# First of two expert mixtures: three passes of fp32r parts for fp32 products, with the weights split by GpSimd and the rows gathered ahead

## The chip, the cores and the metric

One core of one Trainium2 chip. The metric is the device time of one execution in microseconds (us), the median of several runs. The engines are TensorE (PE; its weight loads are shown as PEld), VectorE (DVE), ScalarE (ACT), GpSimd (POOL) and SyncE (SP), which here only issues DMAs.

## What is computed

```python
kv = einsum('bhsd,bhse->bhde', k, v); out = einsum('bhsd,bhde->bhse', q, kv)   # 8 x 8 x 576 x 64
x = out / rms(out) * g_norm                       # as 4608 rows of 512
# first mixture: every row goes to one expert of 8
e_idx = argmax(x @ w_gate); gate_w = softmax(x @ w_gate)[e_idx]; eom = sigmoid(x @ w_output_gate)[e_idx]
for e in range(8):                                # w1[e]: 512 x 1024, w2[e]: 1024 x 512
    out[e_idx == e] = gate_w * eom * (relu(x[e_idx == e] @ w1[e]) @ w2[e])
# second mixture: all pairs (row, expert) by falling score; a row takes the first expert that has
# room (576 rows each), then relu(x @ w21[e]) @ w22[e]
```

Everything is fp32, inputs and output.

## The kernel before

**Attention.** A hand-interleaved schedule over 8 batches of 6 chunks. GpSimd multiplies the rows by the inverse root (L492) and stores them to the DRAM tensor `x_rows`, three chunks at a time (L498).

**Routing.** VectorE finds each row's expert and its slot in a list sorted by expert, in which each expert fills whole tiles of 128 rows (L1040 to L1115); TensorE adds the one-hot lists up (L623). The semaphore `s_route` (L1115) says that `tok_i`, the row numbers of each tile, is there. `T1` = 43 is the greatest count of tiles; on this input the eight experts fill 5, 5, 6, 5, 5, 4, 6 and 5 tiles, and the last two are padding.

**First mixture**, the part that changes. For each tile t:

- GpSimd copies the tile's row numbers (L513), then gathers 128 rows of 520 numbers (512 and the row's factor) into the one buffer `xg` (L516), when the rows before have been turned.
- TensorE, in one step of its loop: the first product of tile t (L633: two halves of 512 columns, four chunks each), the turning of tile t+1's rows (L672, four transposes), the second product of tile t-1 (L686, eight chunks), the turning of tile t's h (L693, eight transposes). An fp32 matmul shows as two records, so a product is 16 records.
- VectorE copies the turned rows and the turned h out of PSUM (L1127, L1132), and scores y of tile t-2 against the second router: eight operations with an accumulator (L1138), one for each expert, `y` times a row of `wg2b`, written to `prod`.
- ScalarE does relu (L855) and the scaling of y by the factor (L863), and issues the store of y to `y_rows`.
- SP loads an expert's weights, 4 MB, into one of two sets when the second product of the expert before the preceding one is done (L410, L411).

The loops are real loops with registers; the set of weights is picked by a register read from `tile_par`.

**Selection and second mixture.** VectorE and TensorE search the thresholds of each expert (L1246, L739), and TensorE works through 40 tiles in three passes of fp32r parts: high times high, low part of the weights times high part of the rows, high times low (L648 in `in_parts`). ScalarE makes the high parts with plain copies (L878, L893, L900), VectorE the low parts by subtraction (L1171, L1177, L1184). None of this changes.

```python
passes = ((acts[0], w[0]), (acts[0], w[1]), (acts[1], w[0]))      # 0: high, 1: low
for i in range(3 * chunks):
    a, b = passes[i // chunks]
    if i == 2 * chunks:
        pe.wait_ge(*low_x)                                        # low part of the rows
    mm = pe.matmul(ps, a[:, i % chunks, :], b[:, i % chunks, cols], ...)
```

Of the kernel before, what the change touches and what calls it, by code (L numbers as in the profile page):

```python
# [30 lines left out]
P = 128  # L31
# [28 lines left out]
def build(nc, q, k, v, g_norm, w_gate, w_og, w1, w2, w_gate2, w21, w22, out, debug=None):  # L60
# [20 lines left out]
    HALF = F // 2  # L81

# [26 lines left out]
    with ExitStack() as ctx:  # L109
# [17 lines left out]
        wg2_rows = nc.dram_tensor("wg2_rows", [1, E, DM], F32, kind="Internal").ap()  # L127
        y_rows = nc.dram_tensor("y_rows", [T1 * P, DM], F32, kind="Internal").ap()
# [38 lines left out]
        gcur = sb("gcur", [P, 1], I32)  # L167
# [42 lines left out]
        s_gc = sem("gather_index")  # L210
        s_xg = sem("rows_gathered")
# [8 lines left out]
        s_yst = sem("y_stored")  # L220
# [25 lines left out]
        with ExitStack() as early:  # L246
            def sbe(name, shape, dt=F32):
                return early.enter_context(nc.sbuf_tensor(name, shape, dt))

            xrow = [sbe(f"xrow{i}", [PT, CT, DM]) for i in range(2)]  # L250
            lgs = sbe("lgs", [PT, G1, 2 * E])
# [6 lines left out]
            kvgb = [sbe(f"kvgb{i}", [P, HP, P + 4 * E]) for i in range(2)]  # L258
            kvT = sbe("kvT", [P, HP, P])
            qT = [sbe(f"qT{i}", [P, HP, PT]) for i in range(2)]  # L260
            sq = [sbe(f"sq{i}", [PT, DM]) for i in range(2)]
            q2 = [sbe(f"q2{i}", [PT, DM]) for i in range(2)]
            lraw = [sbe(f"lraw{i}", [PT, CT, H * 2 * E]) for i in range(2)]
        with ExitStack() as router:
            wg2b = router.enter_context(nc.sbuf_tensor("wg2b", [P, E, DM], F32))
            prod = router.enter_context(nc.sbuf_tensor("prod", [P, E, DM], F32))
            router.enter_context(nc.sbuf_tensor("room_of_routing", [P, 2048], F32))
            wg2_t = router.enter_context(nc.sbuf_tensor("wg2_t", [E, DM], F32))
# [23 lines left out]
        w1_sb = w_sb[:, :, 0:KC * F].rearrange("p u (c f) -> p u c f", c=KC)  # L292
        w2_sb = w_sb[:, :, KC * F:].rearrange("p u (c f) -> p u c f", c=FC)
# [36 lines left out]

        ohb = sb("ohb", [P, T1, P], F16)
        bid = sb("bid", [P, T1, P], F16)
        cmp = sb("cmp", [P, T1, NTH], F16)
        room_n = sb("room_n", [P, P], F16)
        ind = sb("ind", [P, NTH], F16)
        best = sb("best", [P, T1])
        a3 = sb("a3", [P, T1, E])
        b3 = sb("b3", [P, T1, E])
        taken = sb("taken", [P, T1, E])
# [30 lines left out]
        ty_ps = bank[6]  # L370
        l8_ps = bank[7]
# [21 lines left out]

        @block.sync
        def _(sp):
# [13 lines left out]
            def load_weights(n, u, w1_src, w2_src):  # L409
                sp.dma_start(w1_sb[:, u, :, :], w1_src.rearrange("(p c) f -> p c f", c=KC)).then_inc(s_wl, 16)  # L410
                sp.dma_start(w2_sb[:, u, :, :], w2_src.rearrange("(p c) f -> p c f", c=FC)).then_inc(s_wl, 16)  # L411
                sp.wait_ge(s_wl, (n + 1) * 32)
                alone(sp)

            load_weights(0, 0, w1[0], w2[0])
            sp.wait_ge(s_fa, 1)
            load_weights(1, 1, w1[1], w2[1])
            sp.wait_ge(s_route, 1)
            with sp.Fori(1, E // 2) as j:
                for u in range(2):  # L420
                    e = j * 2 + u
                    end = sp.value_load(ends_i[0:1, bass.ds(e - 2, 1)], min_val=1, max_val=T1 + 1)
                    sp.wait_ge(s_l2, end)
                    alone(sp)
                    load_weights(e, u, w1[e], w2[e])
# [30 lines left out]
        def _(pool):  # L456
# [45 lines left out]
            pool.wait_ge(s_fa, 1)  # L502
            for b in range(B):
                pool.dma_start(x_rows[b * S:(b + 1) * S, DM:XW].rearrange("(p c) n -> p c n", c=CT),
                               fac[:, b * CT:(b + 1) * CT, :]).then_inc(s_fst, 16)
            pool.wait_ge(s_wgc, 1)
            pool.dma_start(wg2_rows[0, :, :], wg2_t[:, :]).then_inc(s_wgs, 16)
            pool.wait_ge(s_wgs, 16)
            pool.dma_start(wg2b[:, :, :], wg2_rows[:, :, :].to_broadcast([P, E, DM])).then_inc(s_wgb, 16)


            def gather_x(t):
                pool.tensor_copy(gcur[:, :], tok_i[:, bass.ds(t, 1)]).then_inc(s_gc, 1)  # L513
                pool.wait_ge(s_gc, t + 1)
                alone(pool)
                pool.indirect_dma_start(out=xg[:, :], out_offset=None, in_=x_rows[:, :],  # L516
# [37 lines left out]
        def _(pe):  # L554
# [73 lines left out]
            def first_product(n, w, half):  # L628

                if half == 0:  # L630
                    pe.wait_ge(s_xT, n + 1)
# [746 lines left out]
```

## Time and profile before

| | |
|---|---|
| median of 3 runs | 1592.75 us (1592.34 to 1598.07) |
| profiled execution | 1592.23 us, span 1590.4 us |
| PE busy | 1420.8 us, 89% of the span |
| DVE busy | 896.5 us, 56% |
| ACT, POOL busy | 366.1 us (23%), 236.0 us (15%) |
| chain that ended last | PE 78%, DVE 15% |

The first mixture runs from 240 to 894 us, the second from 974 to the end; between the two lies the first search. The page is one profiled execution. A busy TensorE is not TensorE at its peak, because the records of pipelined matmuls overlap and their ends are modelled; the time of a group of matmuls is read from one start to the next. The idle time of an engine that is not the bottleneck costs nothing.

### The profile page before, as it was taken

Reading aid. Unit: us, or ns where it says so; the run is one execution under the profiler, and the core shown is the slowest. Engines: PE = TensorE matmul, PEld = TensorE weight load, DVE = VectorE, ACT = ScalarE, POOL = GpSimd, SP = SyncE. Lnnn points to the kernel's source line nnn. Section 1 sums busy time; section 2 is a strip of 40 time slices with the busy share of each in tenths; the row PEclk is TensorE's granted clock in tenths of the full one; section 3 lists DMA queues with packets and bytes.
Section 4 is the critical chain, followed back from the end, with each engine's and each line's share of the span. In section 5 each row is a group of like instructions: output and inputs, shape, how many; then the busy total and the mean of one; then the engine's idle time right before and its main releaser. Section 6 shows DMA issues by size and latency. Waiting matters only on the chain.

```text
span 1590.4 us, 25626 instructions
## 1 busy us (share of the span) xinstructions
PE 1420.8 (89%) x9036; PEld 955.4 (60%) x9037; DVE 896.5 (56%) x2207; ACT 366.1 (23%) x647; POOL 236.0 (15%) x264
## 2 busy tenths in 40 slices
PE   5989519999999999999999525999999999999997
PEld 5878414444444444444444324787878777777786
DVE  1666782454554544544545566857676767676531
ACT  1655401111111111111111002242324232323331
POOL 1244431010110110101100001111111111111110
PEclk9999759999999999999999755999999999999999
DMA  9997250130313131331101021414141414141400
GB/s 220 250 269 235 60 199 27 40 139 33 145 33 139 40 132 40 139 126 53 33 33 34 14 92 42 140 31 140 32 140 32 146 29 143 32 140 34 144 31 23
DMA packets 49675, 151.13 MB, mean 95 GB/s; under 512 B 5144, under 2 KB 23784, under 8 KB 47408
## 3 DMA queue, kind: packets, MB, share of 16 engines
q1 hardware_dynamic: 30592, 95.43, 19.9%
q0 software_dynamic: 12800, 43.18, 8.6%
q10 hardware_dynamic: 6192, 11.27, 1.8%
q8 instruction: 61, 1.00, 0.3%
q14 instruction: 30, 0.25, 0.1%
HBM read 119.55 MB, written 30.31 MB: 94 GB/s over the span
## 4 chain that ended last, share of the span: by engine, by line
PE 78%; DVE 15%; issue 4%; DMA 1%; ACT 1%; SPq 0%; DVEq 0%; POOLq 0%; POOL 0%; ACTq 0%
PE bank L648 23%; PE bank L633 19%; PE bank L686 19%; PE bank L739 4%; PE bank L693 4%; PE o_ps L600 2%; PE kv_ps L566 1%; PE bank L672 1%; DMA v_sb<-in_v 1%; PE bank L679 1%; DVE lraw L1032 1%; DVE xrow L999 1%; PE qt_ps L588 1%; DVE cmp L1246 1%; DVE ms L969 1%
## 5 line engine op out<-in xcount | busy, mean ns | idle before, releaser
L633 PE MATMUL bank<-w_sb,xT 128*128 x688 | 305.1, 596 | 1.6 <-DVE xT L1127 1.2
L686 PE MATMUL bank<-w_sb,hT 128*128 x688 | 302.5, 592 | 1.0 <-DVE hT L1132 1.0
L633 PEld LDWEIGHTS bank<-w_sb,xT 128*128 128x128 f32 x688 | 128.4, 192 | 147.8 <-issue 147.8
L686 PEld LDWEIGHTS bank<-w_sb,hT 128*128 128x128 f32 x688 | 127.9, 191 | 145.7 <-issue 145.7
L1138 DVE SCALAR_TENSOR_TENSOR prod<-y,wg2b 128x512 f32<-128x512 f32 x344 | 213.7, 687 | 2.9 <-ACT y L863 2.9
L855 ACT ACTIVATE h<-bank 128x512 f32<-128x512 f32 x166 | 99.2, 598 | 489.7 <-PE bank L633 304.1
L1126 DVE COPY factor<-xg 128x1 f32 (+1 forms) x43 | 6.6, 154 | 287.0 <-PE bank L672 287.0
L531 POOL DMA_INDIRECT xg<-y_rows,gat_i x40 | 44.1, 1103 | 417.6 <-PE bank L679 217.5
L693 PEld LDWEIGHTS bank<-ident,h 128*128 128x128 f32 x664 | 85.6, 192 | 22.5 <-issue 20.2
L863 ACT ACTIVATE y<-bank,factor 128x512 f32<-128x512 f32 x43 | 29.6, 688 | 300.0 <-PE bank L686 300.0
L648 PE MATMUL bank<-w_lo,xT_hi 128*128 128x512 f32 x320 | 94.9, 407 | 0.4 <-DVE w_lo L1184 0.4
L648 PE MATMUL bank<-w_hi,xT_hi 128*128 128x512 f32 x320 | 93.4, 414 | 1.3 <-ACT xT_hi L878 0.8
L513 POOL COPY gcur<-tok_i 128x1 int32 (+1 forms) x43 | 16.4, 382 | 523.7 <-DVE xT L1127 515.6
L693 PE MATMUL bank<-ident,h 128*128 128x128 f32 x664 | 89.7, 279 | 0.2 <-ACT h L855 0.2
L648 PE MATMUL bank<-w_hi,hT_hi 128*128 128x512 f32 x320 | 88.0, 410 | 0.8 <-ACT hT_hi L893 0.8
L648 PE MATMUL bank<-w_hi,xT_lo 128*128 128x512 f32 x320 | 87.6, 395 | 0.0
L1132 DVE COPY hT<-bank 128x512 f32<-128x512 f32 x86 | 55.4, 686 | 54.9 <-PE bank L693 54.8
L648 PE MATMUL bank<-w_hi,hT_lo 128*128 128x512 f32 x320 | 83.4, 399 | 0.0
L648 PE MATMUL bank<-w_lo,hT_hi 128*128 128x512 f32 x320 | 83.3, 398 | 0.0
L739 PE MATMUL bank<-cmp,bid 128*128 128x15 f16 x2752 | 79.8, 171 | 0.0
L900 ACT ACTIVATE w_hi<-w_sb 128x1024 fp32r<-128x1024 f32 x64 | 63.9, 1054 | 63.8 <-SPq L442 63.8
L1184 DVE TENSOR_TENSOR w_lo<-w_sb,w_hi 128x1024 fp32r<-128x1024 f32 x64 | 77.6, 1219 | 0.0
(244 smaller groups left out, 1896.5 us busy)
## 6 DMA issues: line engine op xcount, KB each, us to landing
w_sb<-in_moe_w SPq DMA_DIRECT2D x16, 2048.0 KB, 12.5
w_sb<-in_moe_w SPq DMA_DIRECT2D x64, 512.0 KB
y_rows<-y ACTq DMA_DIRECT2D x43, 256.0 KB, 2.0
k_sb<-in_k SPq DMA_DIRECT2D x16, 576.0 KB, 14.8
v_sb<-in_v SPq DMA_DIRECT2D x16, 576.0 KB, 17.1
q_sb<-in_q SPq DMA_DIRECT2D x8, 1152.0 KB, 20.4
x_rows<-xrow POOLq DMA_DIRECT2D x16, 576.0 KB, 5.9
wg2b<-wg_rows POOLq DMA_DIRECT2D x1, 2048.0 KB, 7.3
```

Source lines behind the costliest of these rows:

```text
L531: pool.indirect_dma_start(out=xgs[w % 2][:, 0:DM], out_offset=None, in_=y_rows[:, :], in_offset=bass.IndirectOffsetOnAxis(ap=gat_i[:, w:w ...
L600: mm = pe.matmul(o_ps[x % 2][0:PT, hp // 2, hp % 2 * (P + 4 * E):(hp % 2 + 1) * (P + 4 * E)], qT[x % 2][:, hp, :], kvgb[e % 2][:, hp, :], ...
L633: mm = pe.matmul(h_ps[half][:, :], xT[:, c, :], w[:, c, half * HALF:(half + 1) * HALF], start=(c == 0), stop=(c == KC - 1))
L648: mm = pe.matmul(ps, a[:, i % chunks, :], b[:, i % chunks, cols], start=(i == 0), stop=(i == 3 * chunks - 1))
L686: mm = pe.matmul(y_ps[:, :], hT[:, i, :], w[:, i, :], start=(i == 0), stop=(i == FC - 1))
L693: mm = pe.transpose(th_ps[half][:, i * P:(i + 1) * P], h[:, half * 4 + i:F:FC], ident[:, :])
L739: mm = pe.matmul(cps[:, 0:NTH], bid[:, g, :], cmp[:, g, :], start=False, stop=(g == T1 - 1))
L855: act.activation(h[:, half * HALF:(half + 1) * HALF], h_ps[half][:, :], ACT.Relu).then_inc(s_h, 1)
L900: act.activation(w_hi[:, u, cols], w_sb[:, u, cols], ACT.Copy).then_inc(s_whi, 1)
L1132: dve.tensor_copy(hT[:, half * 4:(half + 1) * 4, :].rearrange("p a b -> p (a b)"), th_ps[half][:, :]).then_inc(s_hT, 1)
L1138: ch.inc(dve.scalar_tensor_tensor(out=prod[:, e, :], in0=y[:, :], scalar=1.0, in1=wg2b[:, e, :], op0=ALU.mult, op1=ALU.mult, accum_out=sc_ ...
L1184: dve.tensor_tensor(w_lo[:, u, cols], w_sb[:, u, cols], w_hi[:, u, cols].bitcast(F32), ALU.subtract).then_inc(s_wlo, 1)
```

## The change

**Products.** The first mixture uses `in_parts` too. ScalarE makes the high parts of the turned rows and of h, VectorE the low parts (`rows_low`, `hT_low`), by a subtraction of one operand in PSUM and one in SBUF. All loops over the 43 tiles are written out. The score operations write to PSUM (`prod_ps`, two banks in turn), from the third on with a wait for the one before the last.

**Weights.** Expert 0: ScalarE copies (`first_high(0)`) and GpSimd subtracts (`low_piece`), both after the x rows are stored. Expert 1: ScalarE copies after the routing, GpSimd subtracts after ten gathers. Experts 2 to 7: GpSimd does both, after all gathers. A piece is 128 x 1024, eight make an expert. SP loads them by pieces with two in flight.

**Gathers.** Tiles 0 and 1 are gathered into `xg` and `xg2`. The others go into one of three staging buffers, from there to `x_sorted` in DRAM (a store by SP), and from there into `xg` or `xg2` (a load issued by ScalarE, `sorted_in`). The index copy is gone.

**Moved.** The stores of the factor and the turned router go from GpSimd's to SP's queue, and `wg2b` is spread after the routing. `y` is double-buffered. Early buffers are laid out in another order.

```diff
 # SP
+for t in range(2, T1):
+    i, nth = t % STAGED, (t - 2) // STAGED + 1
+    sp.wait_ge(s_xs[i], nth * 16)
+    sp.dma_start(x_sorted[t * P:(t + 1) * P, :], xst[i][:, :]).then_inc(s_xo[i], 16)
+for e in range(2, E):
+    end = sp.value_load(ends_i[0:1, e - 2:e - 1], min_val=1, max_val=T1 + 1)
+    sp.wait_ge(s_l2, end)
+    for i in range(PIECES):
+        wait_pos(sp, s_pl[i % 2], ((e - 2) * (PIECES // 2) + i // 2) * 16)
+        load_piece(e % 2, i, w1[e], w2[e], s_pl[i % 2])
...
 # GpSimd
+def low_piece(u, i):
+    pool.tensor_tensor(w_lo[:, u, cols(i)], w_sb[:, u, cols(i)], w_hi[:, u, cols(i)].bitcast(F32),
+                       ALU.subtract).then_inc(s_split, 1)
...
+for i in range(PIECES):
+    pool.wait_ge(s_fhi, i + 1)
+    low_piece(0, i)
 pool.wait_ge(s_route, 1)
 pool.wait_ge(s_fst, 16 * B)
-gather_x(0)
-with pool.Fori(1, T1) as t:
-    pool.wait_ge(s_xT, t)
-    alone(pool)
+for t in range(10):
     gather_x(t)
+for i in range(PIECES):
+    pool.wait_ge(s_fhi, PIECES + i + 1)
+    low_piece(1, i)
+for t in range(10, T1):
+    gather_x(t)
+for e in range(2, E):
+    for i in range(PIECES):
+        pool.wait_ge(s_pl[i % 2], ((e - 2) * (PIECES // 2) + i // 2 + 1) * 16)
+        pool.tensor_copy(w_hi[:, e % 2, cols(i)], w_sb[:, e % 2, cols(i)]).then_inc(s_phi, 1)
+        pool.wait_ge(s_phi, (e - 2) * PIECES + i + 1)
+        low_piece(e % 2, i)
...
 # TensorE
+rows_in(0)
+for t in range(T1 + 1):
+    if t < T1:
+        w = one_set(w1_both, set_of(t))
+        need = pe.value_load(tile_wait[0:1, t:t + 1], min_val=PIECES, max_val=PIECES * E)
+        pe.wait_ge(s_split, need)
+        for half in range(2):
+            first_in_parts(t, w, half, None, nothing)
+    if t + 1 < T1:
+        rows_in(t + 1)
+    if t > 0:
+        second_in_parts(t - 1, one_set(w2_both, set_of(t - 1)), None, None, nothing)
+    if t < T1:
+        h_turned(t)
...
 # ScalarE
+first_high(0)
+act.wait_ge(s_route, 1)
+act.wait_ge(s_fst, 16 * B)
+first_high(1)
+rows_high(0)
+sorted_in(2)
+for t in range(T1 + 1):
+    if t < T1:
+        relu(t)
+    if t + 1 < T1:
+        rows_high(t + 1)
+    if t + 3 < T1:
+        sorted_in(t + 3)      # waits for s_xo and for s_xlo >= t + 2
+    if t > 0:
+        scaled(t - 1)
+    if t < T1:
+        hT_high(t)
...
 # VectorE
+factor_kept(0)
+rows_low(0)
+for t in range(T1 + 2):
+    if t == 2:
+        dve.wait_ge(s_wgb, 16)
+    if t >= 2:
+        scores(t - 2)
+    if t + 1 < T1:
+        factor_kept(t + 1)
+        rows_low(t + 1)
+    if t < T1:
+        hT_low(t)
```

## Rows read from the trace of the kernel before

**Rows 1.** The page, busy tenths and granted clock in 40 equal slices.
```profile
PE   5989519999999999999999525999999999999997
PEclk9999759999999999999999755999999999999999
```

**Rows 2.** Timeline, TensorE, a tile of the first mixture: start, us, what.
```profile
599.68 7.03 PE L633 MATMUL bank<-w_sb,xT 128*128 x16
...
607.02 7.03 PE L686 MATMUL bank<-w_sb,hT 128*128 x16
...
614.78 7.03 PE L633 MATMUL bank<-w_sb,xT 128*128 x16
```

**Rows 3.** Timeline, TensorE, a tile of the second mixture without a search.
```profile
1537.70 1.18 PE L648 MATMUL bank<-w_hi,xT_hi 128*128 128x512 f32 x4
...
1543.77 2.12 PE L648 MATMUL bank<-w_hi,hT_hi 128*128 128x512 f32 x8
...
1550.27 1.18 PE L648 MATMUL bank<-w_hi,xT_hi 128*128 128x512 f32 x4
```

**Rows 4.** Timeline, VectorE, the same tile of the first mixture.
```profile
608.13 0.68 DVE L1138 SCALAR_TENSOR_TENSOR prod<-y,wg2b 128x512 f32<-128x512 f32 x1
...
612.41 0.69 DVE L1138 SCALAR_TENSOR_TENSOR prod<-y,wg2b 128x512 f32<-128x512 f32 x1
...
614.53 1.29 DVE L1132 COPY hT<-bank 128x512 f32<-128x512 f32 x2 [1.01 <-PE bank L693]
```

**Rows 5.** Timeline, VectorE and GpSimd in attention, from several windows.
```profile
80.02 1.84 DVE L1032 TENSOR_TENSOR lraw<-lraw,rin 96x768 f32<-96x768 f32 x1
81.01 1.75 POOL L492 TENSOR_TENSOR xrow<-xrow,rin 96x512 f32<-96x512 f32 x1
...
182.67 2.05 POOL L492 TENSOR_TENSOR xrow<-xrow,rin 96x512 f32<-96x512 f32 x2
182.77 3.77 DVE L1032 TENSOR_TENSOR lraw<-lraw,rin 96x768 f32<-96x768 f32 x1
...
196.29 0.95 DVE L1032 TENSOR_TENSOR lraw<-lraw,rin 96x768 f32<-96x768 f32 x1
...
200.44 0.72 POOL L498 DMA_DIRECT2D x_rows<-xrow  x1 [0.30 <-POOL xrow L492]
```

**Rows 6.** Two lines alone: durations in ns, min/median/max, first and last start.
```profile
L492 POOL TENSOR_TENSOR xrow<-xrow,rin x48: 1032/1042/1798, 58.9 to 203.2; 96x512 f32<-96x512 f32 x48
...
L999 DVE TENSOR_TENSOR xrow<-o_ps,g_sb x48: 616/686/687, 36.5 to 192.3; 96x512 f32<-96x512 f32 x48
```

**Rows 7.** Timeline, the routing's steps and the first product.
```profile
211.92 0.55 DVE L1075 TENSOR_TENSOR inc<-inc,cnt 96x384 f32<-96x384 f32 x1
...
233.38 0.18 DVE L1115 TENSOR_SCALAR cap_v<-cap_v 128x43 f32<-128x43 f32 x1
...
240.56 9.63 PE L633 MATMUL bank<-w_sb,xT 128*128 x16 [1.24 <-DVE xT L1127]
```

**Rows 8.** ScalarE's weight copy (ns min/median/max); then DMA issues, us to landing.
```profile
L900 ACT ACTIVATE w_hi<-w_sb x64: 1039/1051/1073, 958.9 to 1519.9; 128x1024 fp32r<-128x1024 f32 x64
...
y_rows<-y ACTq DMA_DIRECT2D x43, 256.0 KB, 2.0
...
xg<-x_rows,gcur POOLq DMA_INDIRECT x43, 3.6
```

**Rows 9.** Timeline, SP's issues of weight loads (L410: first mixture, L437: second).
```profile
327.52 0.35 SPq L410 DMA_DIRECT2D w_sb<-in_moe_w  x1
...
402.98 0.34 SPq L410 DMA_DIRECT2D w_sb<-in_moe_w  x1
...
644.47 0.34 SPq L410 DMA_DIRECT2D w_sb<-in_moe_w  x1
...
704.85 0.34 SPq L410 DMA_DIRECT2D w_sb<-in_moe_w  x1
...
1009.09 12.38 SPq L437 DMA_DIRECT2D w_sb<-in_moe_w  x6
```

More of the change, by code:

```diff
@@ L219, in build @@
         s_y = sem("y_ready")
-        s_yst = sem("y_stored")
+        s_yst = [sem(f"y_stored{i}") for i in range(2)]
         s_wgt = sem("router_turned")
@@ L416, in _, with load_piece @@
-            sp.wait_ge(s_fa, 1)
-            load_weights(1, 1, w1[1], w2[1])
-            sp.wait_ge(s_route, 1)
[L419 to L425, printed above, removed]
+            def load_piece(u, i, w1_src, w2_src, s):
+                w, at = (w1_src, i) if i < PIECES // 2 else (w2_src, i - PIECES // 2)
+                sp.dma_start(w_sb[:, u, i * w_piece:(i + 1) * w_piece],
+                             w.rearrange("(p c) f -> p (c f)", p=P)[:, at * w_piece:(at + 1) * w_piece]).then_inc(s, 16)
@@ L539, in scatter @@
                                         in_=ys[w % 2][0:rows, :], in_offset=None).then_inc(s_out[w % 2], 16)
-            pool.wait_ge(s_yst, 16 * T1)
-            pool.wait_ge(s_tx, T1)
+            for i in range(2):
+                pool.wait_ge(s_yst[i], (T1 + 1 - i) // 2 * 16)
+            pool.wait_ge(s_xlo, T1)
             for w in range(NT2):
@@ L625, in _ @@
             mm.then_inc(s_ids, 1)
-            def first_product(n, w, half):
-                if half == 0:
-                    pe.wait_ge(s_xT, n + 1)
-                for c in range(KC):
-                    mm = pe.matmul(h_ps[half][:, :], xT[:, c, :], w[:, c, half * HALF:(half + 1) * HALF],
-                                   start=(c == 0), stop=(c == KC - 1))
-                mm.then_inc(s_l1, 1)
             def in_parts(ps, acts, w, cols, chunks, low_w, low_x, done, point):
@@ L680, in y_rows_in @@
                 mm.then_inc(s_tx, 1)
-            def second_product(n, w):
-                pe.wait_ge(s_hT, n * 2 + 2)
-                wait_pos(pe, s_y, n)
-                for i in range(FC):
-                    mm = pe.matmul(y_ps[:, :], hT[:, i, :], w[:, i, :], start=(i == 0), stop=(i == FC - 1))
-                mm.then_inc(s_l2, 1)
             def h_turned(n):
@@ L1179, in hT_low, with factor_kept, scores @@
                                       ALU.subtract).then_inc(s_hlo, 1)
+            def factor_kept(t):
+                dve.wait_ge(*rows_there(t))
+                ch.inc(dve.tensor_copy(factor[:, t:t + 1], xgs[t % 2][:, DM:DM + 1]))
+                ch.wait()
+            def scores(t):
+                dve.wait_ge(s_y, t + 1)
+                wait_pos(dve, s_sc, t)
+                for e in range(E):
+                    if e >= 2:
+                        dve.wait_ge(s_dve, ch.base + ch.n - 1)
+                    ch.inc(dve.scalar_tensor_tensor(out=prod_ps[e % 2][:, :], in0=ys[t % 2][:, :], scalar=1.0, in1=wg2b[:, e, :],
+                                                    op0=ALU.mult, op1=ALU.mult, accum_out=sc_raw[:, e:e + 1]))
+                ch.wait()
+                dve.tensor_scalar(score[:, t, :], sc_raw[:, :], cap_v[:, t:t + 1], None, ALU.min).then_inc(s_sc, 1)
+            factor_kept(0)
[3 more added lines that the diff above has]
+                    dve.wait_ge(s_wgb, 16)
+                if t >= 2:
+                    scores(t - 2)
[4 more added lines that the diff above has]
+                    hT_low(t)
+            dve.wait_ge(s_sc, T1)
+            ch.inc(dve.memset(taken[:, :, :], 0.0))
+            link(dve.memset(room[:, :], float(CAP)))
             def weights_low(kk, u, i):
```

224 lines of the change are left out of this document (90 added, 134 removed).

## The prediction

> **What bounds the kernel now.** I read the page's slices first: from slice 7 to slice 22 TensorE is busy at 9 tenths, at full granted clock [rows 1]. That stretch is the first mixture, the only part whose arithmetic the change touches. Then the timeline of one of its tiles: the first product starts at 599.68, the second at 607.02 and the next tile at 614.78 [rows 2], so a tile takes 15.10 us and TensorE never stops. A product is 16 matmul records of 0.43 us, two records for each fp32 product of 512 columns. The other engines have room: VectorE's eight score operations start 0.61 us apart (608.13 to 612.41), 4.9 us in all, and its two copies of h take 1.29 us [rows 4]. TensorE sets the end here, until another engine's work per tile passes its own.
>
> **The products.** The second mixture already works in three passes of fp32r parts with the same shapes and transposes. In its last tiles, where no search lies between, the first product starts at 1537.70, the second at 1543.77 and the next tile at 1550.27 [rows 3]: 12.57 us a tile, 2.53 less. The loop over tiles 1 to 42 has 42 such periods: 42 x 2.53 = 106.3 us. Tile 0 begins at a granted clock of 0.5, which is 1.2 GHz: its product takes 9.63 us instead of 7.03 [rows 7]. A record starts every 0.86 us there, so a pass is 0.43; twelve of those 24 passes fill the same slow 5.1 us and the rest take 12 x 0.233, 7.9 in all: 1.7 us less. The last second product gives 24 x 0.233 = 5.6 against 7.0: 1.4. Sum: **-109.4 us**. That is the whole gain, and it holds while the other engines keep to 12.57.
>
> **ScalarE and VectorE per tile.** ScalarE now makes the high parts (three copies moved from VectorE) and issues the load of sorted rows beside the store of y; with relu and y these are six operations on half the columns of one that takes it 1.05 us [rows 8], so under 6.3 us a tile: hidden. VectorE does 4.9 of scores, 1.3 and 0.65 of subtractions and a few small ones, 7.6 us: hidden alone. But its order matters: the scores of t-2 stand ahead of the low part of tile t+1's rows. Without a disturbance that part is ready some 8.8 us into step t; the third pass of tile t+1 asks for it at 12.57 + 1.9 = 14.5. The cover is **5.7 us**. ScalarE waits for the same part before it issues a load, and the y scaling and the high parts of h queue behind that; they have as much cover.
>
> **What GpSimd costs VectorE.** The score operation has two inputs in SBUF, and GpSimd's new work is a copy and a subtraction of 128x1024 for each of eight pieces of an expert. The trace shows what such a pair does: VectorE's product at L1032, 0.95 us alone (196.29), took 1.84 when it came beside the second of three GpSimd products, whose third then took 1.75 instead of 1.03 [rows 5, 6]; and 3.77 when it came just after the first of three (182.77 beside 182.67), so that it waited for all three [rows 5]. VectorE's L999, with one input in PSUM, never took over 0.687 in 48 [rows 6]. So the two exclude each other if both read two SBUF operands, and a run of GpSimd operations can keep VectorE out for its whole length. The Trainium skill, "SBUF — State Buffer", section "Who interferes with whom", says the same of a DVE instruction with two SBUF inputs against a GpSimd one that reads SBUF: the second to issue fully blocks until the first finishes. By that sentence alone the 3.77 would be under 2, and part (d) below would be 11 for each expert and not up to 13; the row decides.
> A subtraction: GpSimd takes 1.03 us for 512 elements [rows 6], so 2.05 for 1024. The copy is nowhere in the trace. Bounds: 1.05 (ScalarE's same copy [rows 8]) and 2.05; I take 1.3, as one input is read and not two. The skill's "GPSIMD Engine Reference", section 3.1, has one-input bodies at 1.03 to 1.8 cycles an element, an estimate of 0.9 to 1.5 us, by which an expert's split would be 27 to 32 us. Between copy and subtraction it waits for itself, 0.3 us (as in the row at 200.44 [rows 5]); a piece is 3.7 us, an expert 30.
>
> **(a) Routing, +15.** Expert 0's eight subtractions stand in GpSimd's stream as soon as the x rows are stored, about 211.5, with nothing between them: 8 x 2.0 = 16 us. Just then VectorE is in its routing chain, from 211.92 (L1075) to 233.38 (L1115) [rows 7], nearly all two-input SBUF operations, and this chain alone sets when TensorE starts. Bounds: 0 (no exclusion) and 16. I take 15, as the run is unbroken like the one that gave 3.77.
> **(b) Start, +2.** After the routing ScalarE first makes expert 1's high parts, 8 x 1.05 [rows 8] = 8.4, then tile 0's: TensorE starts 9 us after the routing instead of 7.0 (233.6 to 240.56 [rows 7]).
> **(c) Expert 2's weights, +16.** All 43 gathers stand ahead of expert 2's split in GpSimd's stream, and all 41 sorted stores ahead of its load in SP's. Counted from the routing's end: gathers 0 to 9 until 17, expert 1's split until 34, then 33 gathers. With three staging buffers each waits for gather and store: 3.6 + 2.0 us [rows 8], about 6.5 with the waits, 2.2 a tile, so until 106; last store and first piece (512 KB each, six issued in 12.4 us [rows 9]) until 115, then the split, 31 us: 146. TensorE wants these weights after ten tiles (experts 0 and 1 have five each: loads at 327.52 and 402.98 are five periods apart [rows 9]): 9 + 10.3 + 9 x 12.57 = 132. It waits 14, and loses 2 more as the clock drops [rows 7]. Bounds: 3 us (copy 1.05, cycle 5.7) and 40 (copy 2.05, cycle 8.5).
> **(d) Experts 3 to 7, +60.** A split begins 11.75 + 4 us after the preceding expert's first product and runs 30 to 37 us. Meanwhile a score operation gets in about once for each GpSimd operation: 0.61 + 1.7 = 2.3 us each, so a tile's eight take 18.5 and VectorE needs 21 us a tile. The first tile hit is 3 us into its scores and ends 2 us too late, the second 9: 11. With one in for each piece it is 12 and 1: 13. I take 12, five times. Bounds: 0 and 18 each.
> Sum: 1592.2 (span 1590.4 and 1.8 around it, within 0.6 of the runs' median 1592.75) - 109.4 + 15 + 2 + 16 + 60 = 1576, say **1575 us**. The gathers themselves, hidden before behind a prefetch, stay hidden: 2.2 us a tile against 12.57, with ScalarE's loads three tiles ahead. Sorted rows written and read again are 22 MB in some 540 us, 41 GB/s, where the weight pieces alone reach 3.1 MB in 12.4 us, 254 GB/s [rows 9].
>
> **Rivals.**
> *VectorE keeps the port.* Its score operations overlap by 0.07 us [rows 4], as GpSimd's do, so a batch of eight might shut GpSimd out. Then a batch loses one wait only, inside the cover, and GpSimd loses 5 us in each 12.57: a split takes 50 and ends 66 us after the preceding expert's start. Five tiles last 62.8, four (expert 5: loads at 644.47 and 704.85 [rows 9]) 50.3: 3 + 3 + 3 + 16, 25 in place of 60: **1541**. Nothing in the trace has such a batch beside GpSimd, for or against.
> *No exclusion that counts*, as the score writes to PSUM now: (a) and (d) vanish, (b) and 12 for (c) stay: 1592 - 109 + 14 = **1497**. Against it: the product at 182.77.
> *GpSimd becomes the bound* (the other side). If the copy costs as much as the subtraction, a piece with two score operations let in is 2.05 + 2.05 + 0.4 + 1.2 = 5.7 us, a split 46, and 15.8 + 46 is all of a five-tile expert; VectorE does two tiles in a split where 3.7 are due. (d) is 17 x 5 = 85, (c) 40: -109 + 15 + 2 + 40 + 85 = +33: **1625**. With (a) to (c) as above it turns slower than before when a split costs over 15 us of TensorE's time.
> *It doesn't do what it says*: the pass rate of 0.233 isn't met with a set picked by a register. The fp32 products pick theirs so already, without a gap [rows 2]: 2 in 100.
>
> **Chances.** Forecast 0.45, VectorE keeps the port 0.22, no exclusion 0.08, GpSimd the bound 0.20, other 0.05. The forecast's own range is 1555 to 1600. The range for 8 in 10 leaves out the 1497 case and the far side of the slow one: **1525 to 1622**. A measurement of this kernel tells about 0.5% from no change, 8 us. Faster: 0.30 of the forecast's 0.45, both fast rivals, a little of the rest: 0.61. Same: 0.12 of the forecast, 0.04 of the slow case: 0.17 with the rest. Slower: 0.03 and 0.16, 0.22 with the rest.
>
> **What would show it.** The tile period in stretches without a split is 12.6; the routing's end (L1115's counterpart) lies 15 us later, with two-input operations of several us beside GpSimd; TensorE has one gap of over 10 us at tile 10, waiting for GpSimd's subtraction, and shorter ones two or three times an expert, waiting for the rows' low part by VectorE; score operations in a split average over 1.5 us. I am wrong if score operations stay at 0.69, if the copy is over 1.6, or if gathers take over 3 us each.

## The result, and the profile after

The changed kernel takes 1603.2 us (median of 8 runs, 1599.0 to 1606.5), the kernel before 1596.6 beside it (8 runs, 1592.3 to 1600.3): ratio 1.0043, 95% interval 1.0024 to 1.0062. So it is slower by 0.4%, inside the 0.5% called no change above, where 1575 was forecast. The profiled execution took 1601.4 us (span 1599.6), against 1592.2 (1590.4).

First the page of the changed kernel: TensorE's busy tenths and granted clock in 40 slices (which answer to [rows 1]), and three groups of its costliest.

```profile
PE   5988416994679797979899525999999999999997
...
PEclk8989757997789898989899856999999999999999
...
L1180 DVE SCALAR_TENSOR_TENSOR bank<-y,wg2b 128x512 f32<-128x512 f32 x344 | 320.4, 1001 | 0.5 <-ACT y L885 0.5
...
L668 PE MATMUL bank<-w_hi,xT_hi 128*128 (+1 forms) x664 | 199.5, 424 | 37.0 <-POOL w_lo L523 34.0
...
L668 PE MATMUL bank<-w_hi,xT_lo 128*128 (+1 forms) x664 | 191.2, 411 | 46.9 <-DVE xT_lo L1159 46.9
```

The unbroken nines of before are gone: one hole in slices 10 and 11, then notches every second slice, each with a lower clock. The last columns of the groups name both: TensorE stood 34.0 us for a subtraction by GpSimd and 46.9 us for the rows' low part by VectorE, whose score operation (L1180) has a mean of 1001 ns where those of [rows 4] take 0.69 us.

The timeline of TensorE, in order: the first product, an undisturbed tile period (answers to [rows 2]), tile 10, the ten waits for the rows' low part (three shown), the last second product.

```profile
254.87 2.07 PE L668 MATMUL bank<-w_hi,xT_hi 128*128 x4 [0.88 <-ACT xT_hi L896]
...
265.73 1.19 PE L668 MATMUL bank<-w_hi,xT_hi 128*128 x4 [0.68 <-issue]
...
278.31 1.17 PE L668 MATMUL bank<-w_hi,xT_hi 128*128 x4
...
413.01 2.07 PE L668 MATMUL bank<-w_hi,xT_hi 128*128 x4 [34.03 <-POOL w_lo L523]
...
444.84 2.08 PE L668 MATMUL bank<-w_hi,xT_lo 128*128 x4 [2.65 <-DVE xT_lo L1159]
...
465.60 2.07 PE L668 MATMUL bank<-w_hi,xT_lo 128*128 x4 [6.49 <-DVE xT_lo L1159]
...
767.11 2.08 PE L668 MATMUL bank<-w_hi,xT_lo 128*128 x4 [7.92 <-DVE xT_lo L1159]
...
894.43 2.13 PE L668 MATMUL bank<-w_hi,hT_hi 128*128 x8 [1.49 <-ACT hT_hi L911]
```

From 265.73 to 278.31 is 12.58 us, so the faster products are there. The waits come in pairs, 2.65 and about 6.4, one pair for each expert from 3 to 7 (the second of the last pair is 7.92); the ten sum to 46.9.

**The ledger**, profiled execution against profiled execution. Attention up to the first step of the routing: -3.4, which moves from run to run (the same step lies between 204.0 and 212.6 in the kernels below that don't touch what stands ahead of it). Routing, from the copy of `tot` to the end of `cap_v`: 40.5 us against 26.2, +14.4. Its end to the first product: 10.3 against 7.0, +3.3. First product to the first mixture's end: 645.5 (254.87 to 900.34) against 653.8 (240.56 to 894.35), -8.3, in which the faster products, the hole at tile 10 and the five splits balance. The rest +3.2. Sum +9.2.

The routing's steps on VectorE (they answer to [rows 7]), and below them GpSimd's subtractions for expert 0, which had begun just before:

```profile
207.95 2.22 DVE L1105 TENSOR_SCALAR cnt<-cnt 128x8 f32<-128x8 f32 x1
...
210.40 2.48 DVE L1107 TENSOR_TENSOR inc<-inc,cnt 96x384 f32<-96x384 f32 x1
212.91 2.59 DVE L1108 TENSOR_TENSOR inc<-inc,onehot 96x384 f32<-96x384 f32 x1
215.53 0.79 DVE L1109 TENSOR_REDUCE slot<-inc 96x48 f32<-96x384 f32 x1
...
217.78 2.26 DVE L1111 TENSOR_SCALAR slot_i<-slot_i 96x48 int32<-96x48 int32 x1
...
244.38 0.18 DVE L1147 TENSOR_SCALAR cap_v<-cap_v 128x43 f32<-128x43 f32 x1
```
```profile
207.77 19.79 POOL L523 TENSOR_TENSOR w_lo<-w_sb,w_hi 128x1024 fp32r<-128x1024 f32 x8 [5.89 <-ACT w_hi L865]
```

L1107 took 0.55 us before. It is in most cases one VectorE operation for one subtraction (eight in 19.79 us; alone 2.35). What I had not seen coming is that operations with a single SBUF tensor are held as well (L1105, L1111), while the reduction isn't.

The next view is the chain that led to the 34 us: the critical pieces between the routing and tile 10 (start, us, what), a part of it.

```profile
266.32 18.87 POOL w_lo L523 x8
285.34 1.23 POOL xst L533
286.88 3.78 DMA xst<-x_rows,tok_i
290.68 4.57 DMA x_sorted<-xst
295.51 1.42 POOL xst L533
297.23 5.05 DMA xst<-x_rows,tok_i
302.30 4.77 DMA x_sorted<-xst
307.33 4.38 DMA xst<-x_rows,tok_i
311.73 4.64 DMA x_sorted<-xst
...
374.22 5.16 DMA xst<-x_rows,tok_i
```

Gather, store, gather, store: each buffer's next gather waits for its last store, and the two together take 7 to 10 us.

And a split with the scores of a tile in it, VectorE and then GpSimd:

```profile
448.87 2.89 DVE L1180 SCALAR_TENSOR_TENSOR bank<-y,wg2b 128x512 f32<-128x512 f32 x1
...
451.68 1.52 DVE L1180 SCALAR_TENSOR_TENSOR bank<-y,wg2b 128x512 f32<-128x512 f32 x1
...
453.13 2.88 DVE L1180 SCALAR_TENSOR_TENSOR bank<-y,wg2b 128x512 f32<-128x512 f32 x1
...
464.85 0.69 DVE L1159 TENSOR_TENSOR xT_lo<-bank,xT_hi 128x512 fp32r<-128x512 f32 x1
```
```profile
448.48 2.72 POOL L523 TENSOR_TENSOR w_lo<-w_sb,w_hi 128x1024 fp32r<-128x1024 f32 x1
451.15 1.50 POOL L551 CAST w_hi<-w_sb 128x1024 fp32r<-128x1024 f32 x1
452.73 2.72 POOL L523 TENSOR_TENSOR w_lo<-w_sb,w_hi 128x1024 fp32r<-128x1024 f32 x1
```

The two engines take turns: a score operation ends 0.5 us after the GpSimd operation it stood behind, and GpSimd's next runs 0.4 us longer than alone (2.34, and 1.04 for the copy). Two score operations go into a piece of 4.25 us, so the eight of a tile last 16 us (448.25 to 464.4) where 5 would do; the low part of the next rows comes at 464.85, and TensorE starts at 465.60.

### The profile page after: what moved, and what is told of

Its sections match the earlier page's. It is cut to its first block, busy times and chain, and to the rows that moved or that the text cites. A ratio compares the mean times of both kernels' runs of the same rounds, so it can differ in the third digit from the quotient of the medians.

```text
span 1599.6 us, 26685 instructions
## 1 busy us (share of the span) xinstructions
PE 1329.6 (83%) x9724; PEld 1093.2 (68%) x9724; DVE 1025.8 (64%) x2207; ACT 447.6 (28%) x792; POOL 429.5 (27%) x323
## 4 chain that ended last, share of the span: by engine, by line
PE 55%; DVE 25%; DMA 8%; issue 5%; POOL 3%; ACT 2%; SPq 0%; ACTq 0%; DVEq 0%; POOLq 0%
PE bank L668 40%; DVE bank L1180 9%; PE bank L748 4%; DMA xst<-x_rows,tok_i 4%; PE bank L706 3%; DMA x_sorted<-xst 3%; POOL w_lo L523 2%; PE o_ps L629 2%; PE kv_ps L595 1%; DMA v_sb<-in_v 1%; PE bank L699 1%; DVE xrow L1031 1%; DVE lraw L1064 1%; PE qt_ps L617 1%; DVE cmp L1269 1%
## 5 line engine op out<-in xcount | busy, mean ns | idle before, releaser
L1180 DVE SCALAR_TENSOR_TENSOR bank<-y,wg2b 128x512 f32<-128x512 f32 x344 | 320.4, 1001 | 0.5 <-ACT y L885 0.5
L668 PE MATMUL bank<-w_hi,xT_hi 128*128 (+1 forms) x664 | 199.5, 424 | 37.0 <-POOL w_lo L523 34.0
L668 PE MATMUL bank<-w_hi,xT_lo 128*128 (+1 forms) x664 | 191.2, 411 | 46.9 <-DVE xT_lo L1159 46.9
L668 PE MATMUL bank<-w_lo,xT_hi 128*128 (+1 forms) x664 | 192.3, 406 | 0.4 <-DVE w_lo L1207 0.4
L668 PEld LDWEIGHTS bank<-w_hi,xT_lo 128*128 128x128 f32 x664 | 128.8, 196 | 81.7 <-DVE xT_lo L1159 51.3
L668 PE MATMUL bank<-w_hi,hT_hi 128*128 (+1 forms) x664 | 179.3, 408 | 2.3 <-ACT hT_hi L911 2.3
L668 PE MATMUL bank<-w_lo,hT_hi 128*128 (+1 forms) x664 | 171.6, 399 | 0.0
L668 PE MATMUL bank<-w_hi,hT_lo 128*128 (+1 forms) x664 | 170.7, 397 | 0.0
L523 POOL TENSOR_TENSOR w_lo<-w_sb,w_hi 128x1024 fp32r<-128x1024 f32 x64 | 164.2, 2575 | 9.8 <-ACT w_hi L865 5.9
L668 PEld LDWEIGHTS bank<-w_lo,xT_hi 128*128 128x128 f32 x664 | 126.3, 194 | 29.2 <-DVE w_lo L1207 0.9
L551 POOL CAST w_hi<-w_sb 128x1024 fp32r<-128x1024 f32 x48 | 63.5, 1324 | 199.6 <-DMA w_sb<-in_moe_w 199.6
## 6 DMA issues: line engine op xcount, KB each, us to landing
q_sb<-in_q SPq DMA_DIRECT2D x8, 1152.0 KB, 18.9
```

Of the source, the lines that this page charges most:

```text
L523: pool.tensor_tensor(w_lo[:, u, cols(i)], w_sb[:, u, cols(i)], w_hi[:, u, cols(i)].bitcast(F32), ALU.subtract).then_inc(s_split, 1)
L551: pool.tensor_copy(w_hi[:, e % 2, cols(i)], w_sb[:, e % 2, cols(i)]).then_inc(s_phi, 1)
L1180: ch.inc(dve.scalar_tensor_tensor(out=prod_ps[e % 2][:, :], in0=ys[t % 2][:, :], scalar=1.0, in1=wg2b[:, e, :], op0=ALU.mult, op1=ALU.mult ...
```

## The experiments

Theory: four things cost what the faster products give, (a) the subtractions of expert 0 in the routing, (b) the start, (c) the late weights of expert 2, (d) score operations that take turns with the splits. Ten kernels, each the changed one with what its diff shows; the kernel before ran beside them (1593.9 to 1595.2).

The stages of every profiled execution, in us, for what follows: the time up to the copy of `tot`; the routing (to the end of `cap_v`); from there to the first product; from there to the start of the last second product, called the mixture; the rest.

| kernel | up to `tot` | routing | start | mixture | rest | span |
|---|---|---|---|---|---|---|
| before | 207.4 | 26.2 | 7.0 | 646.6 | 703.2 | 1590.4 |
| changed | 204.0 | 40.5 | 10.3 | 639.6 | 705.2 | 1599.6 |
| e1 | 211.2 | 40.8 | 10.1 | 612.4 | 705.8 | 1580.3 |
| e2 | 211.6 | 40.8 | 10.3 | 572.5 | 703.8 | 1539.0 |
| e3 | 208.5 | 40.8 | 10.0 | 617.0 | 705.6 | 1581.9 |
| e4 | 210.2 | 27.5 | 10.4 | 639.5 | 704.8 | 1592.3 |
| e5 | 208.8 | 40.8 | 10.3 | 539.1 | 706.8 | 1505.7 |
| e6 | 205.2 | 25.2 | 10.3 | 554.1 | 706.5 | 1501.2 |
| e7 | 212.6 | 25.2 | 6.6 | 560.4 | 706.3 | 1511.0 |
| e8 | 206.7 | 40.5 | 10.2 | 635.1 | 705.8 | 1598.3 |
| e9 | 211.6 | 25.2 | 10.7 | 550.1 | 707.3 | 1504.8 |
| e10 | 205.5 | 25.2 | 10.3 | 550.0 | 704.7 | 1495.6 |

The first column differs by up to 8.6 us between kernels in which nothing ahead of `tot` was edited. So what an edit did is read from its own stages, and a few us between two medians say little.

### e1: expert 2's split ahead of half the gathers

```diff
-            for t in range(10, T1):
+            for t in range(10, 24):
                 gather_x(t)
             for e in range(2, E):
+                if e == 3:
+                    for t in range(24, T1):
+                        gather_x(t)
```

SP's stream is reordered in the same way (store 23, then expert 2's load).

> One change to the changed kernel: expert 2's split stands after gather 23 in GpSimd's stream and its load after store 23 in SP's, not after all 43. The ledger of the changed kernel's profile is: routing +14.4, start +3, one wait of 34 us at tile 10, about 65 us in the five splits of experts 3 to 7. My theory: the wait at tile 10 goes, and expert 2's split now runs beside score operations like the other five and costs TensorE 13: -21, about 1581 us. Rival: the gathers that are left over are the real limit, so that the wait comes back at a later tile (experts 3 or 4, or rows that are not there): no gain, 1600 us, and a wait of 20 to 34 us at another tile.

Measured: 1579.1 us (1574.3 to 1582.3), ratio 0.989 [0.985, 0.993]. The 34 us are gone, and TensorE's wait for the rows' low part grows from 46.9 to 52.8, for now expert 2's split has scores beside it too (a pair of 2.67 and 6.43, while of expert 3's pair one wait of 5.95 is left):

```profile
L677 PE MATMUL bank<-w_hi,xT_hi 128*128 (+1 forms) x664 | 199.7, 425 | 3.3 <-ACT xT_hi L905 1.7 <-issue 1.7
...
L677 PE MATMUL bank<-w_hi,xT_lo 128*128 (+1 forms) x664 | 191.6, 412 | 52.8 <-DVE xT_lo L1168 52.8
```

The mixture is 27.2 us shorter. So the order of the stream is the cause of (c), worth 24 us net in the medians. The place fits these loads: where expert 0 alone had more than 24 tiles, TensorE would need rows that now stand behind expert 2's weights, and these wait for expert 0's end. No run tries that.

### e2: the scores read y from PSUM

```diff
-ch.inc(dve.scalar_tensor_tensor(out=prod_ps[e % 2][:, :], in0=ys[t % 2][:, :], scalar=1.0, in1=wg2b[:, e, :],
+ch.inc(dve.scalar_tensor_tensor(out=prod[:, e % 2, :], in0=y_pss[t % 2][:, :], scalar=factor[:, t:t + 1], in1=wg2b[:, e, :],
```

y alternates between two PSUM banks, for which TensorE's second product of tile t waits for the scores of tile t-2, and the product goes to SBUF.

> One change to the changed kernel: the score operation reads the second product from PSUM (two banks in turn) and scales it itself, so that only one of its inputs lies in SBUF; its output goes to SBUF. My theory (two SBUF inputs against GpSimd's reads): score operations stay near 0.7 us during a split, the five splits cost TensorE under 5 us in all, -60: about 1541 us; the wait at tile 10 and the routing stay. Rival: VectorE is late for another reason (ScalarE's chain of waits, the order of the work, or GpSimd holds up any VectorE operation): score operations stay at over 1.2 us in a split and the time at 1590 or more.

Measured: 1537.8 us (1535.1 to 1540.7), ratio 0.963 [0.960, 0.967]. Groups of the profile:

```profile
L1184 DVE SCALAR_TENSOR_TENSOR prod<-bank,factor,wg2b 128x512 f32<-128x512 f32 x344 | 234.1, 747 | 0.3 <-ACT y L889 0.3
...
L670 PE MATMUL bank<-w_hi,xT_hi 128*128 (+1 forms) x664 | 192.9, 413 | 34.0 <-POOL w_lo L525 31.2 <-ACT xT_hi L900 1.7 <-issue 1.1
...
L670 PE MATMUL bank<-w_hi,xT_lo 128*128 (+1 forms) x664 | 182.8, 397 | 0.0
```

With one input in PSUM the score operation falls from 1001 to 747 ns, GpSimd's copy from 1324 to 1041, and TensorE never waits for the rows' low part. That is (d), with a little of (c): of the 65 us between the medians (67.1 in the mixture), 2.8 are the wait at tile 10, which is 31.2 instead of 34.0. The edit moves the product's output as well. That the output isn't the cause is seen in the routing, where L1107 and L1108 with their output in SBUF are held and L1106 (0.16 us), with one input in PSUM, is not.

### e3: five staging buffers in place of three

```diff
-    STAGED = 3
+    STAGED = 5
```

> One change to the changed kernel: five staging buffers, not three. In its trace three gathers and stores take 8.5 us, 2.85 us a tile (gather about 4.5 to landing, store 3.5). Theory: each transfer's latency is the limit, so five buffers give 1.7 us a tile, 33 gathers 56 us and not 94, and the wait of 34 us at tile 10 all but goes: about 1570 us. Rival: the DMA engines are the limit (busy 77% in that stretch): landings grow with the count in flight, over 2.4 us a tile, and the wait stays over 19 us: 1588 us or more.

Measured: 1583.7 us (1582.6 to 1588.5), ratio 0.993 [0.991, 0.996], between theory and rival. The windows view, of the changed kernel and then of this one (stretch, us, busy time and instructions by engine, clock, DMA share, GB/s):

```profile
300.00:360.00 60.00, 60.00 (x289) 49.72 (x288) 36.20 (x104) 16.71 (x29) 21.88 (x21) 1.00 0.77 231
```
```profile
290.00:345.00 55.00, 55.00 (x266) 45.62 (x265) 31.94 (x91) 14.55 (x26) 27.73 (x28) 1.00 0.94 307
```

Gathers 10 to 42 start every 1.95 us instead of 2.78. Two more buffers to three are 67% more and brought 43% more gathers; the DMA engines are now busy 94% of the time instead of 77%. TensorE still waits 6.6 us at tile 10, and expert 2's split, which begins 29 us sooner after the routing's end, now meets scores and costs a wait of 2.68 of its own. So with three buffers the number in flight set the cycle. That with five it is the DMA engines is my reading of the 94%; no run tests it.

### e4: zeros in place of expert 0's low parts

```diff
-                low_piece(0, i)
+                pool.memset(w_lo[:, 0, cols(i)].bitcast(F32), 0.0).then_inc(s_split, 1)
```

> One change to the changed kernel: GpSimd fills the low part of expert 0's weights with zeros in place of the eight subtractions (that part of expert 0's products is left out). It writes SBUF and reads nothing. Theory (VectorE's two-input operations wait for GpSimd's reads): the routing operations with two SBUF inputs, 2.5 us and more in the changed kernel, are back at 0.55 to 0.9; those with one input that were stretched too (a tensor_scalar 0.39 to 2.22, a cast 0.59 to 2.23) may still wait for the fills. Routing ends 10 to 14 us earlier, the time is about 1588. Rival: any GpSimd instruction shuts VectorE out: two-input operations are stretched by one fill each.

Measured, a single run: 1594.1 us, where the theory said 1588. VectorE in the routing:

```profile
214.15 0.76 DVE L1105 TENSOR_SCALAR cnt<-cnt 128x8 f32<-128x8 f32 x1
...
215.13 0.56 DVE L1107 TENSOR_TENSOR inc<-inc,cnt 96x384 f32<-96x384 f32 x1
...
217.70 0.91 DVE L1111 TENSOR_SCALAR slot_i<-slot_i 96x48 int32<-96x48 int32 x1
...
237.50 0.18 DVE L1147 TENSOR_SCALAR cap_v<-cap_v 128x43 f32<-128x43 f32 x1
```

From the copy of `tot` (210.21) it is 27.5 us, against 40.5 and, before the change, 26.2. All 13 us reach the end of the mixture, which is as long as in the changed kernel; what is missing in the time stands ahead of `tot`. Beside fills, which read nothing, two-input operations run at their own time, while L1105 and L1111 still stretch. So there are two kinds of exclusion. Some 8 of the 14.4 us of (a) are two-input operations (L1107, L1108, L1117 and one of L1120, 2 us each) and go by what GpSimd reads. The other 6 are casts and `tensor_scalar` with one tensor; they shrink too, but a fill is also shorter than a subtraction (eight take 7.5 us and not 19.8), and this run doesn't part the two. The Trainium skill, "SBUF — State Buffer", section "Who interferes with whom", has both: two SBUF inputs contend with a GpSimd operation that reads, and copy, cast and `tensor_scalar` can take a two-port mode that contends with any; `tensor_reduce` never contends. The rows agree for two inputs, for `tensor_scalar`, for casts (L1110, 0.51 us beside fills and 0.27 before) and for the reduction L1109 (0.79 and 0.81).

### e5: e1 and e2 together

The two diffs above in one kernel.

> The edits of the two earlier runs together: score operations that read PSUM, and expert 2's split after gather 23. The routing is left as in the changed kernel. My theory (the two prices are separate; the score's exclusion made the early split cost 13, which goes too): against the run with score operations from PSUM alone another 31 to 34 less, 1505 us, no wait of over 3 us at tile 10. Rival: with a split beside the running tiles something else appears (ScalarE's chain, DMAs): 1515 or more.

Measured: 1508.0 us (1506.0 to 1510.1), ratio 0.945 [0.943, 0.948]. They add up: from 1603 it is 24 and 65 and another 6, the waits for the rows' low part that e1 had added (46.9 to 52.8) and that are gone here. In the mixture it is 100.5 for 27.2 and 67.1. What is left of the bill is (a) and (b).

### e6: expert 0's subtractions behind the routing

```diff
+            pool.wait_ge(s_route, 1)
+            pool.wait_ge(s_fst, 16 * B)
+            for t in range(3):
+                gather_x(t)
             for i in range(PIECES):
                 pool.wait_ge(s_fhi, i + 1)
                 low_piece(0, i)
-            pool.wait_ge(s_route, 1)
-            pool.wait_ge(s_fst, 16 * B)
-            for t in range(10):
+            for t in range(3, 10):
```

On top of e5; tile 0's first pass waits for the high parts only, its second for the low parts.

> As the run with both edits, and expert 0's eight subtractions stand after the routing and three gathers in GpSimd's stream; TensorE's first tile waits for the low part of w1's four pieces only before its second pass. Theory: the routing is 14 us shorter, as nothing stands beside VectorE there, and TensorE's start loses 1 to 3 of it: 12 less, about 1493. Rival: the subtractions now stand before the start itself (8 x 2.4 us), and the start loses all that the routing gains: 1502 to 1508.

Measured: 1503.7 us (1499.6 to 1505.0), ratio 0.942 [0.939, 0.945]. The routing takes 25.2 us, the full 15.6 less, and the mixture takes 15.0 more than in e5: nearly all of it is given back, and in the profiles the 4 us between the two kernels stand ahead of `tot` (205.2 against 208.8). The time is the rival's, with more places than the start to lose it in. VectorE shows the largest, 5.9 us (TensorE waits for the low part made at 290.86):

```profile
278.76 0.09 DVE L1198 DVE_READ_ACCUMULATOR prod<-bank,factor,wg2b 128x1 f32 x1
278.88 11.89 DVE L1201 TENSOR_SCALAR score<-sc_raw,cap_v 128x8 f32<-128x8 f32 x1
...
290.69 0.14 DVE L1189 COPY factor<-xg 128x1 f32<-128x1 f32 x1
290.86 0.69 DVE L1177 TENSOR_TENSOR xT_lo<-bank,xT_hi 128x512 fp32r<-128x512 f32 x1
```
```profile
271.97 18.76 POOL L531 TENSOR_TENSOR w_lo<-w_sb,w_hi 128x1024 fp32r<-128x1024 f32 x8
```

An operation on eight elements a partition, 0.23 us alone, stood 11.9 us, to the very end of expert 1's eight subtractions. The other waits are 1.6 and 1.2 for the subtractions themselves, and 3.0 for rows whose gather stands behind them: 11.7 with the 5.9. Some 3 us more go in passes at the lower clock behind the two longest (1.87 us apart at 291.61, 0.93 where undisturbed).

### e7: the start relieved

```diff
-            sp.dma_start(wg2b[:, :, :], wg2_rows[:, :, :].to_broadcast([P, E, DM])).then_inc(s_wgb, 16)
...
                 sort_out(t)
+                if t == 3:
+                    sp.dma_start(wg2b[:, :, :], wg2_rows[:, :, :].to_broadcast([P, E, DM])).then_inc(s_wgb, 16)
```

On top of e6, the 2 MB spread of `wg2b` is so issued behind two sorted stores, and ScalarE turns tile 0's rows ahead of expert 1's copies.

> As the run before, and the start is cleared: the spreading of the second router's weights (2 MB) stands after two sorted stores in SP's queue, and ScalarE turns tile 0's rows before it copies expert 1's weights. In the changed kernel the first product starts 10.3 us after the routing's end where it was 7.0: the first gather landed 8 us after its issue and not 3.5, beside those 2 MB. Theory: 3 to 4 us less than the run before, about 1489. Rival: the first gather's landing isn't due to the 2 MB: no change over 1 us.

Measured: 1511.8 us (1507.7 to 1513.4), ratio 0.947 [0.944, 0.949], 8 us more than e6. The theory fails on the time. The first product comes 6.6 us after the routing instead of 10.3, and the two first gathers land 3.5 us after their issue instead of 6.9, so the spread and the copies were what made (b); the run moves both and doesn't part them. But pass 2 then waits 5.3 us for the subtractions, and the same 128x8 operation stood 13.4 us, which cost TensorE 7.4: the mixture is 6.3 us longer than in e6. From the routing's end on that is 2.6 us more. In the profiles the rest of the 8 stands ahead of `tot` (212.6 against 205.2), where nothing was edited; its cause is open.

### e8: the order on ScalarE

```diff
-                if t + 3 < T1:
-                    sorted_in(t + 3)
                 if t > 0:
                     scaled(t - 1)
                 if t < T1:
                     hT_high(t)
+                if t + 3 < T1:
+                    sorted_in(t + 3)
```

On the changed kernel alone.

> One change to the changed kernel: in ScalarE's stream the load of sorted rows of tile t+3, which waits for VectorE's low part of tile t+1, stands behind the scaling of y and the high parts of h and not ahead of them. In the changed kernel's splits VectorE has about 2.3 us of idle time after each late low part, while ScalarE does y and h. Theory A (that chain is a part of the 65 us): 2.3 us twice an expert go, 15 to 23 less, about 1582. Theory B (only the shared port counts; GpSimd's work fills the gap): less than 5 us.

Measured: 1604.2 us (1600.1 to 1608.0), ratio 1.006 [1.004, 1.008]: no change beside 1603.2, as in theory B. In the trace TensorE's waits for the rows' low part are 40.5 us instead of 46.9, and the mixture is 4.4 shorter. So ScalarE's wait behind the same low part, named in the prediction, is worth some 4 us of (d) in the one profile there is, too little for the medians to show.

### e9 and e10: a gap between subtractions

e9 is e6 with `for t in range(5)` ahead of expert 0's subtractions. e10 adds a wait of GpSimd for its own last subtraction, for experts 0 and 1:

```diff
                 pool.wait_ge(s_fhi, PIECES + i + 1)
+                pool.wait_ge(s_split, PIECES + i)
                 low_piece(1, i)
```

> The kernel of e6 with five gathers, not three, ahead of expert 0's subtractions in GpSimd's stream. In e6 (1503.7) ScalarE waited 10 us for the sorted rows of tile 3, whose gather stood behind the subtractions, and TensorE lost 3.0 us of it; and at tile 3 TensorE waited 5.9 us, since VectorE's last operation of a tile's scores (128x8, 0.23 us alone) took 11.89 us beside an unbroken run of five of expert 1's subtractions. Theory A, the order of the gathers is what is left: the 3.0 goes, the second pass of tile 0 waits 2.5 us longer for the subtractions, the 5.9 stays or goes with the place at which expert 1's split falls: 1498 to 1503. Rival B, what is given back moves on once more, as from e5 to e6: 1504 or more.

> As e9, and GpSimd waits for each of its subtractions for experts 0 and 1 before it issues the next, as it does in the later splits by the wait between copy and subtraction. Theory A, an unbroken run keeps VectorE out until its end (11.89 us in e6, 5.12 us at the end of expert 1's split in the changed kernel), and a gap of 0.06 us lets one operation in each time: no VectorE operation with two operands in SBUF takes over 3 us in either split, and the time is e9's or up to 6 us less. Rival B, VectorE gets in by chance or by its own timing and the gap changes nothing: operations of 5 to 12 us beside these subtractions stay possible, and TensorE's wait at tile 3 stays as in e9.

Measured: 1502.4 us (1500.8 to 1506.5), ratio 0.942 [0.939, 0.944], and 1498.7 (1494.6 to 1503.4), ratio 0.940 [0.937, 0.943]. The 128x8 operation in e9, and then in e10:

```profile
282.97 9.87 DVE L1201 TENSOR_SCALAR score<-sc_raw,cap_v 128x8 f32<-128x8 f32 x1
```
```profile
278.11 2.40 DVE L1203 TENSOR_SCALAR score<-sc_raw,cap_v 128x8 f32<-128x8 f32 x1
```

In both it fell in expert 1's split. Without a gap it stood to the split's end (282.97 + 9.87 = 292.84; the split is 274.00 to 292.80), with one it stood behind one subtraction, and TensorE's wait of 3.9 us there is gone. Theory A holds for the single operation, seen once in each kernel, and no VectorE operation in either split of e10 took over 2.4 us (most of them read one input from PSUM, so this is the only one that was put to the test). The time is another matter: the mixture is 550.0 us against 550.1 in e9. Pass 2 waits 4.7 us for the subtractions instead of 3.7, the next wait for them is 1.5 instead of 0.5, and expert 3's split, behind gathers 24 to 42, now ends too late and costs 2.9. The 3.7 us between the two medians, whose ranges overlap, are not shown to come from the gaps; in the profiles the difference stands ahead of `tot` and behind the mixture. The price of the gaps is 1.3 and 1.4 us a split (19.90 and 20.24 against 18.59 and 18.80). The theory for e9 holds for its time too: the mixture is 4.0 us shorter than in e6, though pass 2 now waits 3.7 us for the subtractions. e10 has the lowest median of this study, 6.0% under the kernel before.

## Why the prediction was wrong

**The products, right.** -109.4 rests on 12.57 us a tile; undisturbed tiles show 12.58 and 12.53. First product to the first mixture's end is -8.3; without the two terms measured below, 36 and 63, that is -107, 2 short of the forecast. Tile 0's step is a part of it: 10.86 us against 11.88, 1.0 less where the sum had 1.7.

**(a) Routing, right:** +14.4 for 15. The reason was half the story: only two-input operations were thought to be held, but L1105, L1111 and L1113 with one tensor took 2.2 us each; and of the large one-hot products, two-input operations too, all but the first two (L1117 and L1120) came after the subtractions' end (227.56).

**(b) Start, +3.3 for 2.** ScalarE's eight copies were counted, the DMA side was not: tile 0's rows landed 8 us after their issue, beside the 2 MB spread that now starts at the same moment. In e7, without the spread there, they land in 3.5.

**(c) Expert 2's weights, the step that failed:** +36 for 16. By its own steps, from the routing's end: expert 1's split ended at 40.8 and not 34 (gathers 0 to 9 took 21.7 us for 17, with rounds of 8.9 and 7.7 between the threes; then eight subtractions took 18.9 for 17). The 33 gathers took 89.8 us and not 72, 2.72 each. Last gather to first piece 9.6, for 9. The split 28.0, for 31. Sum 168 for 146; TensorE asked at 134.4, for 132; it waits 34 for 14, and loses 2 by the clock in both. So the weights came 22 us late and TensorE 2 us late, and 18 of it are the gather cycle of the 33: 3.6 + 2.0 and a little were taken from [rows 8], where one gather at a time runs in an idle queue. With three in flight, the store beside them and the sorted loads, gather and store took some 4.6 and 3.8, and the cycle 8.2. The far bound (8.5) was the right value; the row chosen was of an unloaded queue, although the change was what loads it. The prediction had set the traffic at 41 GB/s, by spreading 22 MB over the 540 us of the whole mixture; the gathers and stores run in its first 120 us, at 231 GB/s from 300 to 360.

**(d) Experts 3 to 7, nearly right:** 63 for 60. From tile 10's first product to the last second product, 413.01 to 894.43, there are 33 periods and 481.4 us; 33 x 12.57 is 414.8, which leaves 66.6, and 1.7 go off, since the last product stands 2.5 us behind the start of its transposes (891.90) where a tile's first product stands 0.8 (277.50 to 278.31). Another 2.1 go off for the slower passes right behind the hole at tile 10, which are in (c). (The 65 in the expectation of e1 had these 2 in it.) Of the 63, 46.9 are TensorE's waits and 16 what the clock costs after the ten: the passes at 444.84 start 1.87 and 1.55 us apart, where undisturbed ones start 0.93 apart. The pair was forecast as 2 and 9 late and is 2.65 and in most cases 6.4: a score operation costs 2.13 us, not 2.3. The clock's share had been left out of this term, and the two errors nearly cancel. The piece of a split came out by luck as well: 3.7 us from a copy of 1.3, a subtraction of 2.05 and a wait of 0.3, where the rows have 1.04, 2.34 and 0.07.

**The sum.** 20 for (c), 3 for (d), 2 for the products and 1 for (b), less 1 for (a), are the 25 us between the sum of 1576 and the profiled 1601. The direction was wrong because a net gain of 17 us stood on a cost of 93: a fifth more of the cost turns the sign. The time lay in the range, and that it depends on one cycle time could have been read off the bounds of (c), whose far end alone gives 1599.

**The rivals.** "VectorE keeps the port" falls with the rows at 448.87: the two take turns. "No exclusion" falls by the score operations of 1.52 and 2.88 us, and by e2. "GpSimd becomes the bound" has the right sign and the wrong mechanism: the copy is 1.04 us, not 2.05, and a split beside scores lasts 32.5 us (431.41 to 463.9), not 46. Two sums are off by a little and decide nothing: with expert 2's six tiles a split that ends 66 us after its start costs nothing, so the first rival has 3 + 3 + 16 = 22 and not 25; and the estimate of 27 to 32 us for a split adds up to 26 to 31 by its own terms.

## What to carry to other kernels

Price a DMA cycle by rows with the same number of transfers in flight; a latency read from an idle queue is only the near bound. When work goes to GpSimd, list VectorE's operations beside it by what they read: here moving one operand to PSUM was worth 65 us, four times the whole forecast gain. A shared in-order stream needs its parts in order of due time. Read a gain from the stage that was edited: of the 15.6 us that e6 saved in the routing, 15.0 came back in the mixture, while the medians showed a gain of 4.

## What the runs showed of the hardware

**A run without gaps keeps VectorE out for more than one operation.** Beside a run of eight subtractions whose inputs were ready, an operation stood 9.87, 11.89 and 13.44 us (e9, e6, e7), and a score operation of the changed kernel 5.12 us, each to the run's end. With a wait on the engine's own last operation it took 2.40 (e10, once). The 3.77 in [rows 5] fits the same reading, and so does the kernel before at 201.07, against a run of three:

```profile
201.07 3.58 DVE L1045 TENSOR_TENSOR oh<-oh,rank 96x384 f32<-96x384 f32 x1
```
```profile
201.18 3.04 POOL L492 TENSOR_TENSOR xrow<-xrow,rin 96x512 f32<-96x512 f32 x3
```

In the routing and in the splits with a wait between copy and subtraction it was one GpSimd operation at a time (1.5 to 2.9 us). The Trainium skill, "SBUF — State Buffer", section "Summary: rules for kernel authors", has the second to issue wait until the first finishes. The rows agree for the single turns and not for the runs. Why VectorE got its turns in the routing, beside an equally unbroken run, stays open.

**Small operations are held like large ones.** The operation of 128x8 elements takes 0.23 us alone and 11.89 held.

**GpSimd.** The subtraction of 128x1024 fp32 takes 2.34 us alone where twice the product of 512 [rows 6] gives 2.06; the copy takes 1.04. Undisturbed score operations start 0.61 us apart with all in SBUF [rows 4], 0.65 with the result in PSUM (430.46, 431.11, 431.76), and 0.67 with y in PSUM: the PSUM operand costs 10% where nothing is shared, and saves a quarter of the mean over all 344 in a kernel where GpSimd is busy.
